# Attention, routed experts and a dense MLP on one core: two reorderings, in the attention loop and at the entry of the dense stage

## The chip, the cores and the metric

The kernel runs on one core of a Trainium2 chip. The core has a matrix engine (TensorE, PE in the profile, with its weight loads listed apart as PEld), a vector engine (VectorE, DVE), a scalar engine (ScalarE, ACT), a general engine (GpSimd, POOL) and a queue engine that only issues transfers (SyncE, SP). Each runs its own instruction stream in order, and they meet at semaphores. The metric is the device time of one execution in microseconds (us), the median over several.

## The reference

Three stages follow one another. Inputs and outputs are float32.

```python
# attention: 4 batches, 8 heads, 576 positions, head size 64; blockwise causal mask, blocks of 64
scores = q @ k.T / 8; scores = where(block_i >= block_j, scores, -1e9)
attn = exp(scores - max); attn = attn / (sum(attn) + 1e-9); out = attn @ v
x = out laid out as [2304 tokens, 512]

# routed experts: 8 experts of width 1024, one per token, tokens with x @ w_skip <= 0 pass unchanged
e = argmax(x @ w_gate); gate = softmax(x @ w_gate)[e]
x[active] = x + gate * (relu(x @ w1[e]) @ w2[e])

# dense MLP, width 2048
h = x @ w_in; g = max(h, 0) + alpha * min(h, 0); result = g @ w_out
```

## The kernel before, in words

**Attention** handles two heads at a time, a "pair": 16 pairs, numbered n. Pair 0 and pair 15 stand apart, pairs 1 to 14 are seven turns of a hardware loop with two pairs each. The 576 query rows of each head are cut into four tiles of 128 and a tail of 64; the two tails of a pair share one tile. So a pair has nine score units, c = 0 to 8: units 0 to 3 are the first head's tiles with 128, 256, 384 and 512 keys, units 4 to 7 the second head's, and unit 8 is the joint unit (JOINT) with both tails and 576 keys.

One unit passes through this chain: `scores` on PE (L640, JOINT L634, ending with a mask matmul L642), `maxima` on DVE (L981), `exps` on ACT (L849, followed by an accumulator read; `p_done` rises when both are done), `probs_t` on PE (transposes of the probabilities, L652), `pt_out` on DVE (copies them to SBUF, L992 and L989). Score units share three PSUM banks (0, 1, 2), so a score unit waits until the exps of the unit last in its bank are done: unit 1 of the next pair and unit 8 use bank 1, and unit 8 follows unit 6 there.

For the pair behind, n-1, three more pieces of work are placed among the units by number: `probs_v` (the value block, PE L662 and L668) at PV_AT, its evacuation `o_out` on ACT (L854, L856) at O_AT, `to_rows` (the row block, PE L685: it turns the output to token rows and adds the routing logits in the same matmuls) at ROWS_AT, and on DVE `x_out`, `x_tail_out` and `logits_part` (L1016 to L1041), which write the rows. For the pair ahead, n+1, five q/k chunks are transposed on PE (`qk_chunk`, L612 and L616) and evacuated on ACT (`qk_next`, L835 to L840) one unit later, at the units in QK_AT. Chunks and probability transposes use three PSUM banks in turn, in the order of ORDER, so each waits for the evacuation three places back. The lists before:

```python
QK_AT = [1, 2, 3, 5, 7]
PV_AT, O_AT, ROWS_AT, SUMS_AT = 0, 2, 2, 1
```

Every score unit is issued two units ahead of its transposes. SP runs one in-order queue per pair (`load_step`): load q and k of pair n+2 when the split of the pair before is done, load v of pair n when the value block of n-1 is done, `swap` (four transfers of q_t between partition halves, the first two once chunks 0 and 1 are evacuated, the next two after chunk 3; unit 0 of the next pair waits for the first two), two stores of zeros, and in pairs 1 to 8 two weight loads. POOL splits q and k into a rounded part and a rest.

**Experts.** Tokens are scattered by expert with indirect transfers (POOL L524), run through the two products in tiles of 128, and the results stored to `y_slots`.

**Dense MLP.** Six steps (c) of 384 tokens, three token tiles each. POOL gathers the three tiles' expert results (`gather`, L560), DVE adds them, times the gate, to the residual (`u_rows`, L1206), PE transposes by feature block (`u_transposes`, L781), ACT rounds (`u_out`, L946) and DVE takes the rest (`u_parts`, L1212), each for one feature block of 384 tokens through two banks. Then `hidden` (L793) and `project` (L804) follow for 16 blocks f of the width. In the first step all this stands in front of the first matmul; in later steps it lies beside work. Before the first gather POOL waits for the last store and runs a tiny operation on one column (L552). After the first gather POOL loads and splits w_out beside the first step.

## Time and profile before

| | |
|---|---|
| runs of the kernel before | 936.2, 937.68, 938.81 us; median 937.68 us |
| profiled execution | 941.46 us, of which the span is 939.6 us |
| busy share of the span | PE 89%, PEld 77%, DVE 46%, ACT 28%, POOL 26% |
| attention | from 15.8 us (first score unit) to 268.6 us (last row block) |
| router and scatter | to about 307 us |
| experts | to about 497 us |
| dense MLP | from 516.15 us (first product) to the end |
| granted TensorE clock | 0.96 of full in 24 to 285 us, 0.53 in 497 to 516 us, 1.00 from 585 us |

Matmul records overlap, since they include the time in which a matmul fills and drains the array, and their ends are modelled; the weight-load row (PEld) shows when the next matmul's weights go in. A wait is printed in brackets behind the row it held up, with the instruction that ended it. In the listings of waits, the columns are who waited, for whom, the sum in us, how many times, and the longest.

### The profile page before, as it was taken

The numbers are of one execution on the slowest core, as the hardware profiler recorded it, in microseconds if no ns is written. First come the engines' busy times: TensorE is split into PE (matmuls) and PEld (weight loads), VectorE is DVE, ScalarE is ACT, GpSimd is POOL, SyncE is SP. The second block draws the span as 40 slices with busy tenths as digits, with TensorE's granted clock in tenths as the row PEclk, the third lists the DMA queues.
The fourth block names the chain that finished last, engine by engine and source line by source line (L and its number), as shares of the span: only waits on it lengthen the run. The fifth ranks groups of instructions, "written<-read, shape, count | busy, mean of one in ns | idle before, by whom it ended". The sixth has DMA issues, their size and how long they took to land.

```text
span 939.6 us, 15516 instructions
## 1 busy us (share of the span) xinstructions
PE 832.4 (89%) x5243; PEld 723.7 (77%) x5244; DVE 432.3 (46%) x895; ACT 262.4 (28%) x643; POOL 243.4 (26%) x194
## 2 busy tenths in 40 slices
PE   4799999999930789999991999999999999999997
PEld 4577777777720688999981988998988998998996
DVE  2466566667671251232434464344353443443432
ACT  3355555556540221211321111111111112112111
POOL 4422333423007373330266891000001001000000
PEclk8899999999985798999996899999999999999999
DMA  4389899776304493541853320100100101100001
GB/s 113 71 228 244 244 229 260 173 193 166 115 7 184 165 369 114 184 174 45 302 211 90 101 68 0 67 0 12 56 0 17 50 0 28 39 0 12 23 1 33
DMA packets 97620, 103.06 MB, mean 110 GB/s; under 512 B 64320, under 2 KB 64320, under 8 KB 97088
## 3 DMA queue, kind: packets, MB, share of 16 engines
q1 hardware_dynamic: 89984, 74.50, 27.9%
q0 software_dynamic: 4448, 15.73, 5.6%
q10 hardware_dynamic: 3168, 12.58, 3.6%
q8 instruction: 11, 0.18, 0.1%
q14 instruction: 9, 0.07, 0.0%
HBM read 64.78 MB, written 27.53 MB: 98 GB/s over the span
## 4 chain that ended last, share of the span: by engine, by line
PE 71%; DVE 7%; POOL 6%; issue 6%; DMA 5%; SPq 3%; ACT 1%; DVEq 1%; ACTq 0%; POOLq 0%
PE bank L793 21%; PE bank L804 21%; PE bank L751 6%; PE bank L765 6%; PE bank L662 4%; PE bank L652 3%; PE bank L640 2%; PE bank L634 2%; PE bank L685 2%; POOL x_slots L524 2%; DVE neg_max L981 2%; DMA stage<-in_moe_w_in_dram 1%; DMA w_sb<-in_moe_w_dram 1%; POOL wi_lo L537 1%; PE bank L781 1%
## 5 line engine op out<-in xcount | busy, mean ns | idle before, releaser
L1220 DVE TENSOR_SCALAR g_sb<-bank,alpha_sb 128x384 f32<-128x384 f32 x96 | 59.3, 618 | 217.8 <-PE bank L793 217.3
L952 ACT CAST g_hi<-g_sb 128x384 fp32r<-128x384 f32 x96 | 49.5, 515 | 321.6 <-DVE g_sb L1222 321.6
L793 PE MATMUL bank<-u_hi,wi_hi 128*128 128x384 f32 x384 | 130.5, 340 | 1.2 <-DVE u_lo L1212 1.2
L793 PE MATMUL bank<-u_hi,wi_lo 128*128 128x384 f32 x384 | 130.5, 340 | 0.0
L793 PE MATMUL bank<-u_lo,wi_hi 128*128 128x384 f32 x384 | 130.0, 339 | 0.0
L804 PE MATMUL bank<-wo_lo,g_hi 128*128 128x512 f32 x288 | 113.8, 395 | 0.0
L804 PE MATMUL bank<-wo_hi,g_lo 128*128 128x512 f32 x288 | 113.5, 394 | 0.0
L804 PE MATMUL bank<-wo_hi,g_hi 128*128 128x512 f32 x288 | 112.7, 391 | 0.6 <-DVE g_lo L1226 0.6
L751 PEld LDWEIGHTS bank<-rows_t,w_sb 128*128 128x128 f32 x832 | 96.9, 195 | 2.6 <-DVE rows_t L1151 1.5
L751 PE MATMUL bank<-rows_t,w_sb 128*128 128x128 f32 x832 | 97.2, 279 | 1.1 <-DVE rows_t L1151 1.1
L849 ACT ACTIVATE p_sb<-bank,neg_max 128x128 f32<-128x128 f32 (+2 forms) x144 | 79.7, 554 | 61.7 <-DVE neg_max L981 61.5
L981 DVE TENSOR_REDUCE neg_max<-bank 128x1 f32<-128x128 f32 (+2 forms) x144 | 73.7, 512 | 41.1 <-PE bank L634 19.7
L992 DVE COPY p_t<-bank 128x128 f32<-128x128 f32 (+3 forms) x128 | 60.8, 476 | 50.6 <-PE bank L652 50.6
L640 PE MATMUL bank<-k_t,q_t 128*128 128x128 f32 (+3 forms) x256 | 71.3, 365 | 11.4 <-DMA alpha_sb<-in_moe_alpha_dram 5.3
L793 PEld LDWEIGHTS bank<-u_hi,wi_hi 128*128 128x128 f32 x384 | 73.1, 190 | 5.2 <-DVE u_lo L1212 1.6
L652 PE MATMUL bank<-ident,p_sb 128*128 128x128 f32 x400 | 73.4, 289 | 4.1 <-DVE p_t L992 2.1
L560 POOL DMA_INDIRECT u_sb<-y_slots,from_i x18 | 19.1, 1059 | 221.9 <-PE bank L781 217.8
L793 PEld LDWEIGHTS bank<-u_lo,wi_hi 128*128 128x128 f32 x384 | 72.9, 190 | 3.6
L793 PEld LDWEIGHTS bank<-u_hi,wi_lo 128*128 128x128 f32 x384 | 72.9, 190 | 0.0
L492 POOL TENSOR_TENSOR parts<-qk_nat,zero_c 128x512 fp32r<-128x512 f32 (+1 forms) x30 | 33.7, 1145 | 146.4 <-DMA qk_nat<-in_k_dram 146.4
L804 PEld LDWEIGHTS bank<-wo_lo,g_hi 128*128 128x128 f32 x288 | 54.0, 188 | 11.6
L804 PEld LDWEIGHTS bank<-wo_hi,g_hi 128*128 128x128 f32 x288 | 54.1, 188 | 10.2 <-issue 1.2
(143 smaller groups left out, 1286.2 us busy)
## 6 DMA issues: line engine op xcount, KB each, us to landing
w_sb<-in_moe_w_dram ACTq DMA_DIRECT2D x6, 2048.0 KB, 7.9
w_sb<-in_moe_w_dram SPq DMA_DIRECT2D x6, 2048.0 KB, 9.2
q_t<-q_t SPq DMA_DIRECT2D x64, 160.0 KB, 2.5
w_sb<-in_moe_w_dram SPq DMA_DIRECT2D x16, 512.0 KB, 6.3
x_slots<-x_tok SPq DMA_DIRECT2D x14, 512.0 KB, 3.3
y_slots<-x_tok SPq DMA_DIRECT2D x14, 512.0 KB, 4.9
qk_nat<-in_q_dram SPq DMA_DIRECT2D x32, 128.0 KB, 4.4
qk_nat<-in_k_dram SPq DMA_DIRECT2D x32, 128.0 KB, 3.0
```

Source lines behind the costliest of these rows:

```text
L640: pe.matmul(a[:, 0:keys], q_t[:, par, z, h, P * (i + 1):P * (i + 2)], k_t[:, par, h, 0:keys], start=z == 0, stop=False)
L652: last = pe.transpose(t[:, P * j:P * j + P], p_sb[:, c % PB, P * j:P * j + P], ident[:])
L662: last = pe.matmul(O_MAIN[HALF * h:HALF * h + HALF, P * unit:MAIN], v_nat[:, unit, h, :], p_t[:, h, unit, P * unit:MAIN], start=unit == 0, ...
L751: last = pe.matmul(HIDDEN[c][:, P * z:P * z + P], w1_sb[:, par, j, P * f:P * f + P], rows_t[:, j, :], start=j == 0, stop=j == KD - 1)
L765: last = pe.matmul(RESULT, h[:, f, :], w, start=f == 0 and z == 0, stop=f == KF - 1 and z == 2)
L793: last = pe.matmul(dst, w[:, j, P * f:P * f + P], u[:, j, :], start=z == 0, stop=z == len(terms) - 1)
L804: last = pe.matmul(YBANK[i][:, :], g[:, f % GB, P * i:P * i + P], w[:, f, :], start=f == 0 and z == 0, stop=f == FI - 1 and z == 2)
L849: act.activation(p_sb[:, c % PB, 0:keys], scores_ap(c), ACT.Exp, bias=neg_max[:, c:c + 1], accum_out=row_sum[:, par, i, h:h + 1]).then_inc ...
L952: act.copy(g_hi[:, f % GB, :], g_sb[:, f % 2, :]).then_inc(g_hi_done, 1)
L981: dve.reduce_max(neg_max[:, c:c + 1], scores_ap(c), AX.X, negate=True).then_inc(max_done, 1)
L992: dve.tensor_copy(p_t[:, h, 0:i + 1, P * i:P * i + P], t[:, 0:P * (i + 1)].rearrange("p (j c) -> p j c", c=P)).then_inc(pt_evac, 1)
L1220: dve.tensor_scalar(g, a, 0.0, alpha_sb[:, f:f + 1], ALU.min, ALU.mult).then_inc(neg_done, 1)
```

## The change

In attention, the row block moves from unit 2 to the front of unit 8 (JOINT), on PE and on DVE. Score unit 3 moves from unit 1 to unit 0, in front of the value block, so that unit 0 issues two score units and unit 1 none. The q/k chunks move: chunk 0 from unit 1 to 2, chunk 1 from 2 to 3, chunk 4 from 7 to 6. The sums move from unit 1 to 0. The row block's banks are now read by DVE until shortly before the next value block writes them, so `probs_v` gets a wait on `head_part_done`, which starts at one.

At the entry of the dense stage, the first chunk is handled by token tile: each gathered tile has its own semaphore, DVE adds it as soon as it is there, PE transposes its four feature blocks into a bank of its own, and ACT and DVE evacuate that bank whole. The wait for the input weights' split now stands behind the transposes. The tiny POOL operation becomes a semaphore increment.

```diff
-        QK_AT = [1, 2, 3, 5, 7]
-        PV_AT, O_AT, ROWS_AT, SUMS_AT = 0, 2, 2, 1
+        QK_AT = [2, 3, 3, 5, 6]
+        PV_AT, O_AT, SUMS_AT, ROWS_AT = 0, 2, 0, JOINT
+        AHEAD = {c: [c + 2] for c in range(UNITS)}
+        AHEAD[PV_AT], AHEAD[PV_AT + 1] = [2, 3], []
+        UFIRST = [bank[1], bank[2], bank[5]]
...
-            pool.tensor_tensor(zero_c[:], zero_c[:], zero_c[:], ALU.add).then_inc(all_stored, 1)
+            pool.sem_inc(all_stored, 1)
...
-                                            ).then_inc(gathered, 16)
+                                            ).then_inc(gathered if c else first_gathered[i], 16)
...
                 pe.wait_ge(pt_evac, UNITS * n + JOINT)
+                pe.wait_ge(head_part_done, n + 1)
...
             def pair(n, par, first=False, last=False):            # PE
                 for c in range(UNITS):
-                    if c + 2 < UNITS:
-                        scores(c + 2, n, par, first)
-                    elif not last:
-                        scores(c + 2 - UNITS, n + 1, 1 - par, False)
+                    if c == ROWS_AT and not first:
+                        to_rows(n - 1)
+                    for u in AHEAD[c]:
+                        if u < UNITS:
+                            scores(u, n, par, first)
+                        elif not last:
+                            scores(u - UNITS, n + 1, 1 - par, False)
                     if c == PV_AT and not first:
                         probs_v(n - 1)
-                    if c == ROWS_AT and not first:
-                        to_rows(n - 1)
                     probs_t(c, n, last)
...
+            def first_transposes():
+                for i in range(CH):
+                    pe.wait_ge(u_ready, i + 1)
+                    for j in range(KD):
+                        last = pe.transpose(UFIRST[i][:, P * j:P * j + P], u_sb[:, i, P * j:P * j + P], ident[:])
+                    last.then_inc(u_tr, 1)
...
+            first_transposes()
             pe.wait_ge(wi_split, KD)
-            u_transposes(0)
...
             def pair(n, par, first=False, last=False):            # DVE
                 for c in range(UNITS):
+                    if c == ROWS_AT and not first:
+                        x_out(n - 1)
+                        x_tail_out(n - 1)
+                        logits_part(n - 1)
...
-                    if c == ROWS_AT and not first:
-                        x_out(n - 1)
-                    if c == ROWS_AT + 1 and not first:
-                        x_tail_out(n - 1)
-                        logits_part(n - 1)
...
+            dve.sem_inc(head_part_done, 1)
...
+            def first_row(i):
+                dve.wait_ge(first_gathered[i], 16)
+                dve.scalar_tensor_tensor(u_sb[:, i, :], u_sb[:, i, :], gate[:, i:i + 1], x_tok[:, i, :], ALU.mult, ALU.add
+                                         ).then_inc(u_ready, 1)
+            def first_part(i):
+                dve.wait_ge(u_hi_done, i + 1)
+                dve.tensor_tensor(u_lo[:, :, P * i:P * i + P], UFIRST[i][:].rearrange("p (j n) -> p j n", j=KD),
+                                  u_hi[:, :, P * i:P * i + P].bitcast(F32), ALU.subtract).then_inc(u_lo_done, 1)
...
-            u_rows(0)
-            u_parts(0)
+            first_row(0)
+            first_row(1)
+            first_part(0)
+            first_row(2)
+            first_part(1)
+            first_part(2)
```

ACT's `first_out` copies each of the three banks to `u_hi` the same way, and the semaphore counts of the later steps are shifted to match.

TensorE in the loop, from the score unit behind JOINT's to the next: L640 (now L645) are score units, L652 (now L657) transposes of probabilities, L616 a q/k chunk, L685 (now L691) the row block. Before:

```order
L623 ISA
L629 ISA
L640 MATMUL bank<-k_t,q_t 128x128 x2
L642 MATMUL bank<-mask_r,mask_l 128x64
L650 REGISTER_ALU
L652 MATMUL bank_4<-ident,p_sb 128x128 x4
L603 REGISTER_ALU
L616 MATMUL bank<-ident,parts 128x128 x4
L640 MATMUL bank_2<-k_t,q_t 128x256 x2
L642 MATMUL bank_2<-mask_r,mask_l 128x64
L650 REGISTER_ALU
L652 MATMUL bank_4<-ident,p_sb 128x128 x5
```

After:

```order
L647 MATMUL bank<-mask_r,mask_l 128x64
L608 REGISTER_ALU
L655 REGISTER_ALU
L657 MATMUL bank<-ident,p_sb 128x128 x4
L680 ISA
L691 ISA
L691 MATMUL bank<-w_route,o_t 128x146 x5
L645 MATMUL bank_2<-k_t,q_t 128x256 x2
L647 MATMUL bank_2<-mask_r,mask_l 128x64
L608 REGISTER_ALU
L655 REGISTER_ALU
L657 MATMUL bank_4<-ident,p_sb 128x128 x5
```

The chunk is gone from between unit 7's transposes and score unit 1 of the next pair (128x256), and the row block stands there instead.

ScalarE in the loop from the exponentials of unit 3 to those of unit 5: L849 (now L864) are exponentials, L835 to L840 (now L850 to L855) evacuate q/k chunks. Before:

```order
L838 ACTIVATE q_t<-bank_4 128x512
L845 REGISTER_ALU
L849 ACTIVATE p_sb,row_sum<-bank,neg_max 128x512
L831 REGISTER_ALU
L835 ACTIVATE q_t<-bank_4 128x2x64
L836 CAST k_t<-bank_4 128x2x64
L845 REGISTER_ALU
L849 ACTIVATE p_sb,row_sum<-bank_2,neg_max 128x128
L831 REGISTER_ALU
L840 CAST k_t<-bank 128x512
L845 REGISTER_ALU
L849 ACTIVATE p_sb,row_sum<-bank_2,neg_max 128x256
```

After:

```order
L864 ACTIVATE p_sb,row_sum<-bank,neg_max 128x512
L846 ISA
L853 ACTIVATE q_t<-bank 128x512
L860 REGISTER_ALU
L864 ACTIVATE p_sb,row_sum<-bank_2,neg_max 128x128
L846 REGISTER_ALU
L850 ACTIVATE q_t<-bank_4 128x2x64
L851 CAST k_t<-bank_4 128x2x64
L846 REGISTER_ALU
L855 CAST k_t<-bank 128x512
L860 REGISTER_ALU
L864 ACTIVATE p_sb,row_sum<-bank_2,neg_max 128x256
```

The first three chunks stood in front of unit 3, between 3 and 4, and between 4 and 5. Now the first stands between 3 and 4, and the other two together between 4 and 5.

VectorE at the entry of the dense stage: u_sb are the rows, u_lo the rests. Before:

```order
L1189 CAST wi_hi<-wi_raw 128x2048
L1192 TENSOR_TENSOR wi_lo<-wi_raw,wi_hi 128x2048 x2
L1206 SCALAR_TENSOR_TENSOR u_sb<-u_sb,gate,x_tok 128x512 x3
L1212 TENSOR_TENSOR u_lo<-bank_4,u_hi 128x384 x4
L1242 UNCONDITIONAL_BRANCH
```

After:

```order
L1211 CAST wi_hi<-wi_raw 128x2048
L1214 TENSOR_TENSOR wi_lo<-wi_raw,wi_hi 128x2048 x2
L1220 SCALAR_TENSOR_TENSOR u_sb<-u_sb,gate,x_tok 128x512 x2
L1225 TENSOR_TENSOR u_lo<-bank_2,u_hi 128x4x128
L1220 SCALAR_TENSOR_TENSOR u_sb<-u_sb,gate,x_tok 128x512
L1225 TENSOR_TENSOR u_lo<-bank_2,u_hi 128x4x128
L1225 TENSOR_TENSOR u_lo<-bank,u_hi 128x4x128
```

The first rest is taken before the third tile's rows, and each rest spans one token tile and four feature blocks.

## Rows read from the trace of the kernel before

**Rows 1.** Waits of the weight loader in attention, 18 to 285 us.

```profile
PEld bank L634 <- ACT p_sb L849: 10.3, 15, 1.3
...
PEld bank L640 <- ACT p_sb L849: 6.3, 14, 0.5
...
PEld bank L652 <- ACT p_sb L849: 2.9, 14, 0.2
PEld bank L652 <- DVE p_t L992: 2.2, 3, 1.4
```

**Rows 2.** One pair's timeline, TensorE: start us, length us, engine, line, what, [idle, releaser].

```profile
204.77 0.20 PEld L662 LDWEIGHTS bank<-p_t,v_nat 128*64 128x64 f32 x4
...
209.21 1.30 PEld L685 LDWEIGHTS bank<-w_route,o_t 128*128 128x128 f32 x10
...
214.89 1.32 PEld L634 LDWEIGHTS bank<-k_t,q_t 128*128 128x128 f32 x8 [0.64 <-ACT p_sb L849]
214.89 1.55 PE L634 MATMUL bank<-k_t,q_t 128*128 128x512 f32 x8 [0.40 <-ACT p_sb L849]
...
216.53 0.30 PEld L640 LDWEIGHTS bank<-k_t,q_t 128*128 128x128 f32 x2
...
218.16 0.30 PEld L640 LDWEIGHTS bank<-k_t,q_t 128*128 128x128 f32 x2 [0.47 <-ACT p_sb L849]
```

**Rows 3.** The same timeline, ScalarE.

```profile
211.32 0.28 ACT L835 ACTIVATE q_t<-bank 128x128 fp32r<-128x128 f32 x1 [0.82 <-PE bank L612]
...
212.51 0.59 ACT L840 CAST k_t<-bank 128x512 fp32r<-128x512 f32 x1 [0.40 <-PE bank L616]
...
212.99 0.48 ACT L849 ACTIVATE p_sb<-bank,neg_max 128x256 f32<-128x256 f32 x1
...
214.16 0.58 ACT L849 ACTIVATE p_sb<-bank,neg_max 128x384 f32<-128x384 f32 x1 [0.60 <-DVE neg_max L981]
...
214.64 0.19 ACT L849 ACTIVATION_READ_ACCUMULATOR p_sb<-bank,neg_max 128x1 f32 x1
```

**Rows 4.** The same timeline, VectorE.

```profile
211.57 0.56 DVE L1016 TENSOR_TENSOR x_tok<-bank,inv_sum 128x384 f32 x1
...
213.37 0.29 DVE L1041 TENSOR_TENSOR head_part<-bank,inv_sum 128x54 f32 x2
213.59 0.54 DVE L981 TENSOR_REDUCE neg_max<-bank 128x1 f32<-128x384 f32 x1
```

**Rows 5.** Busy time by stretch: length, PE, PEld, DVE, ACT, POOL, clock, DMA share, GB/s.

```profile
124.20:139.30 15.10, 14.30 (x121) 11.30 (x121) 9.92 (x28) 8.68 (x28) 4.76 (x4) 1.00 0.93 237
...
199.84:214.89 15.05, 14.30 (x122) 11.30 (x122) 9.83 (x29) 8.63 (x27) 5.13 (x5) 1.00 0.66 172
```

**Rows 6.** The same timeline as rows 2, SP's swap transfers.

```profile
212.03 4.61 SPq L362 DMA_DIRECT2D q_t<-q_t  x4
```

**Rows 7.** The 64 swap transfers, from issue to landing.

```profile
DMA to landing us min/median/max: 2.4/2.5/4.3
```

**Rows 8.** Timeline of VectorE before the dense stage.

```profile
496.28 4.49 DVE L1192 TENSOR_TENSOR wi_lo<-wi_raw,wi_hi 128x2048 fp32r<-128x2048 f32 x2
508.40 2.86 DVE L1206 SCALAR_TENSOR_TENSOR u_sb<-u_sb,gate,x_tok 128x512 f32<-128x512 f32 x3 [7.63 <-DMA u_sb<-y_slots,from_i]
```

**Rows 9.** Timeline of GpSimd, same place.

```profile
497.52 1.11 POOL L552 TENSOR_TENSOR zero_c<-zero_c 128x1 f32<-128x1 f32 x1 [9.31 <-DMA y_slots<-y_sb]
498.90 2.79 POOL L560 DMA_INDIRECT u_sb<-y_slots,from_i  x1 [0.28 <-POOL zero_c L552]
502.00 0.95 POOL L560 DMA_INDIRECT u_sb<-y_slots,from_i  x1 [0.30 <-issue]
```

**Rows 10.** Chain that ended last, at the scatter: start us, us, what.

```profile
281.27 2.85 POOL x_slots L524
```

**Rows 11.** Timeline of TensorE, same place as rows 8.

```profile
511.41 1.51 PE L781 MATMUL bank<-ident,u_sb 128*128 128x128 f32 x6 [17.21 <-DVE u_sb L1206]
...
516.15 0.69 PE L793 MATMUL bank<-u_hi,wi_hi 128*128 128x384 f32 x1 [1.16 <-DVE u_lo L1212]
```

More of the change, by code:

```diff
@@ L229, in program @@
         gathered = sem("gathered")
+        first_gathered = [sem(f"first_gathered{i}") for i in range(CH)]
         u_ready = sem("u_ready")
@@ L557, in gather @@
                 if c:
-                    pool.wait_ge(u_tr, KD * c)
+                    pool.wait_ge(u_tr, CH + KD * (c - 1))
                 for i in range(CH):
@@ L689, in pair @@
                 for c in range(UNITS):
-                    if c + 2 < UNITS:
-                        scores(c + 2, n, par, first)
-                    elif not last:
-                        scores(c + 2 - UNITS, n + 1, 1 - par, False)
+                    if c == ROWS_AT and not first:
[5 more added lines that the diff above has]
+                            scores(u - UNITS, n + 1, 1 - par, False)
                     if c == PV_AT and not first:
                         probs_v(n - 1)
-                    if c == ROWS_AT and not first:
-                        to_rows(n - 1)
                     probs_t(c, n, last)
-                    if c in QK_AT and not last:
-                        j = QK_AT.index(c)
-                        if j == 0:
-                            pe.wait_ge(split_done, n + 2)
-                        qk_chunk(j, 1 - par, ring("qk", j, n, last))
+                    for j, at in enumerate(QK_AT):
+                        if at == c and not last:
+                            if j == 0:
+                                pe.wait_ge(split_done, n + 2)
+                            qk_chunk(j, 1 - par, ring("qk", j, n, last))
             pe.wait_ge(const_ready, 1)
@@ L772, in _ @@
                 tiles(2 * e2 + 1, 1, e2)
+            def first_transposes():
[4 more added lines that the diff above has]
+                    last.then_inc(u_tr, 1)
             def u_transposes(c):
[L776 removed]
+                pe.wait_ge(u_ready, CH + c)
                 for j in range(KD):
                     if j >= 2:
[L779 removed]
+                        pe.wait_ge(u_lo_done, CH + KD * (c - 1) + j - 1)
                     for i in range(CH):
@@ L789, in hidden @@
                 if f == 0:
-                    pe.wait_ge(u_lo_done, KD * c + KD)
+                    pe.wait_ge(u_lo_done, CH + KD * c)
                 terms = [(w, u, j) for j in range(KD) for w, u in ((wi_hi, u_hi), (wi_hi, u_lo), (wi_lo, u_hi))]
@@ L865, in pair @@
                         o_out(n - 1)
-                    if c - 1 in QK_AT and not last:
-                        qk_next(QK_AT.index(c - 1), n, par)
+                    for j, at in enumerate(QK_AT):
+                        if at == c - 1 and not last:
+                            qk_next(j, n, par)
             act.wait_ge(const_ready, 1)
@@ L940, in _, with first_out @@
             act.copy(wi_hi[:, KD - 1, :], wi_raw[:, KD - 1 - LATE, :]).then_inc(late_hi, 1)
+            def first_out():
+                for i in range(CH):
+                    act.wait_ge(u_tr, i + 1)
+                    act.copy(u_hi[:, :, P * i:P * i + P], UFIRST[i][:].rearrange("p (j n) -> p j n", j=KD)).then_inc(u_hi_done, 1)
             def u_out(c):
                 for j in range(KD):
-                    act.wait_ge(u_tr, KD * c + j + 1)
+                    act.wait_ge(u_tr, CH + KD * (c - 1) + j + 1)
                     act.copy(u_hi[:, j, :], UBANK[j % 2][:, 0:CT]).then_inc(u_hi_done, 1)
@@ L969, in _ @@
             act.sem_inc(out_stored, 16)
-            u_out(0)
+            first_out()
             with act.Fori(0, T_TILES // CH - 1) as c:
@@ L1052, in pair @@
                 for c in range(UNITS):
-                    if c + 2 < UNITS:
-                        maxima(c + 2, n)
-                    elif not last:
-                        maxima(c + 2 - UNITS, n + 1)
+                    if c == ROWS_AT and not first:
+                        x_out(n - 1)
+                        x_tail_out(n - 1)
+                        logits_part(n - 1)
+                    for u in AHEAD[c]:
+                        if u < UNITS:
+                            maxima(u, n)
+                        elif not last:
+                            maxima(u - UNITS, n + 1)
                     if c == SUMS_AT and not first:
```

8 lines of the change are left out of this document (3 added, 5 removed).

## The prediction

> **What bounds the kernel.** I read the busy shares first (PE 89%, the others far below), then the chain that ended last, then the waits of PE in each stage, then one pair's timeline on all engines. In attention, TensorE is the engine that everything else follows, but it does not run without a break. The weight loader waits there for exponentials 43 times, 19.5 us, and three times for VectorE's copies, 2.2 us: 21.7 us in all [rows 1]. Three of these waits come back in every pair: 0.64 us before the joint unit's scores (they need unit 6's exponentials), 0.47 us before unit 1 of the next pair (it needs the joint unit's), and about 0.2 us before unit 5's transposes [rows 1, 2]. A pair takes 15.05 us [rows 5], so without them it would take 13.75.
>
> How much such a wait costs is itself a choice. The record of the joint unit's first matmul shows an idle time of 0.40 us, its weight load 0.64 us [rows 2]. The matmul records include the time to drain, and in a stream without waits the next weight load starts before they end, so I count the weight loader's gap. The Trainium skill (Perfetto Trace Analysis, Identifying the Most-Contended Engine) says the same: matmul busy time is a bad measure, the weight loads' is a good one. By matmul records the waits would be worth only some 12 us.
>
> At the entry of the dense stage TensorE stands still from the last expert tile to 516.15 us, but for twelve transposes. There the chain is what counts: last gather, rows, transposes, rounding, rests.
>
> **Attention, wait by wait.** I set time zero at the value block's first weight load, 204.77 us [rows 2]. The work on TensorE is the same; only the order differs.
>
> *Unit 1 of the next pair.* Before, it came 0.47 us too early [rows 2]. Now the row block stands in front of it (1.30 us of weight loads, [rows 2]), while chunk 4 has been moved ahead. ScalarE evacuates chunk 4 before it takes the joint unit's exponentials, which moves these about 0.5 us later. 1.30 less 0.5 is more than 0.47 by 0.3, so the wait goes, with little to spare.
>
> *Joint unit.* Before, unit 6's maximum started at 213.59 us, right behind the last of the rows' steps on VectorE (213.37 and 0.29 more), and its exponentials started when it was done [rows 3, 4]. That work has moved away, so the maximum starts as soon as unit 6's scores are there, some 0.3 to 0.6 us earlier. What comes last next is ScalarE itself: between the end of chunk 0 on TensorE and the joint unit, it has chunk 0, unit 4, chunk 1, chunk 2, unit 5 and unit 6 to do. By the lengths 0.59, 0.28 twice, 0.59, 0.57 and 0.67 [rows 3], with 0.47 taken for unit 4 and about 0.1 of overlap at each joint (212.51 plus 0.59 against a next start at 212.99), that is 3.1 to 3.2 us. TensorE has in the same stretch what it had before from the row block's end (209.21 + 1.30 = 210.51) to 214.89, 4.38 us, less the waits of 0.84 and less three transposes of unit 2 (0.34 by my reading of the pitch): 3.2 us. About 0.3 of this passes before chunk 0's records end. So ScalarE is late by 0.2 to 0.3 us, spread over unit 5's transposes and the joint unit. I take 0.25 us for each of 14 pairs: 3.5 us. Between its bounds (no wait, or a handover more per chunk, 0.8 us) this is nearest to the rows.
>
> *The new wait of the value block.* VectorE's four row results take 0.56 to 0.27 us each ([rows 4], first and last of them), 1.4 us in all and about 1.2 with their overlap. They start when the row block's records end, and TensorE has unit 1's scores, five transposes and two score units to do meanwhile, over 2 us. It costs nothing, with some 0.5 us of cover. Behind it on TensorE everything would be held up. VectorE's next maximum (unit 1) and the joint copy come about 1.2 us later; TensorE needs the first only behind the value block, 3 us later, and the second for the value block's tail.
>
> *The swap transfers.* Before, the first two were issued at 212.03 us [rows 6], 7.26 after zero. With 0.6 us to the second and 2.5 us to landing [rows 7] they were there at 10.4, and unit 0 of the next pair came at 11.76 (216.53, [rows 2]). Now chunk 1 is evacuated at about 6.0, the transfers issue at about 6.3 and land at 9.4, and unit 0 comes at about 9.8. The slack falls from 1.4 to 0.4 us. In pairs 1 to 8 the transfer engines are 93% busy, against 66% later [rows 5], and SP reaches the swaps later, since loading q, k, v and weights fills its queue. I take 0.3 us of wait for each of the eight, 2.4 us, between 0 and the whole gain.
>
> *The last pair* has no chunks. Its wait for VectorE before the joint transposes (the longest, 1.4 us, [rows 1]) is covered by the row block, its joint unit waits less (about 0.5 us left), but the last value block now waits for the row results, which have only five transposes in front of them: 1.0 us. Left over: 1.5 us. Pair 0 ends in a wait for small loads; I count nothing there, and take 0.5 us out of the 21.7.
>
> Sum: 21.2 - 3.5 - 2.4 - 1.5 = 13.8 us.
>
> **The entry of the dense stage.** Before: the three tiles were there at 508.40 us, the first product started at 516.15, 7.75 us later [rows 8, 11]. Now, behind the last tile: one row step (0.95, a third of 2.86, [rows 8]), four transposes (two thirds of the 1.51 us that six took, [rows 11]), one rounding of 512 columns (0.59, as for a chunk, [rows 3]), one rest (0.75, estimated by the same width) and handovers of 0.3: 3.6 us. Tiles 0 and 1 come 1.5 us and more earlier, one after another, and are through before. Gain 4.1 us.
>
> The gathers start earlier too. The tiny POOL operation took 1.11 us and the first gather 2.79, against 0.95 for the next one; both ended 0.1 and 0.9 us after one of VectorE's two splits (496.28 to 500.77, [rows 8, 9]). The same shows at the scatter, 2.85 us beside a split [rows 10]. So an indirect transfer's issue waits until VectorE's two-input operation ends. Without the tiny operation the first gather gets in at 498.6, the second at 500.8, and the third is issued 1.25 us earlier. Gain 1.2 us. The Trainium skill (SBUF — State Buffer, Who interferes with whom) says that a tensor_tensor does not stall descriptor writing, only GpSimd's reads; the rows show the stall all the same. By that rule the gain would be the tiny operation's 1.4 us, nearly the same.
>
> The clock of the first products stays low as before (0.69 us for the first, [rows 11]), since TensorE has been idle just as long. Dense gain: 5.3 us, between 3 (rows held up by GpSimd's w_out splits) and 6.5. After that TensorE is busy, w_out's splits are far ahead, and the rest shifts.
>
> **Sum.** 13.8 + 5.3 = 19.1 us, from 941.46 to 922.4 for the profiled execution. The timed median before is 937.68, 3.8 us lower; with the same difference 918.6 us.
>
> **Rivals.**
> 1. *Transfers set pairs 1 to 8.* For: 93% busy at 15.05 us per pair [rows 5]; the same bytes in 14.0 us leave no air. Against: q and k are loaded two pairs ahead. Then 8 times 0.75 us is not gained: 924.6 us.
> 2. *Two chunks in a row on ScalarE.* The joint unit waits 0.8 us instead of 0.25 in 14 pairs. For: the evacuation of chunk 0 ends just when chunk 2 needs its bank. Against: ScalarE is idle a third of a pair. 926.3 us. About the same would come out if matmul records were the right measure.
> 3. *The third tile's rows come behind GpSimd's first split of w_out*, which took 1.6 us: it would cost about 1.6 us, 920.2 us. The Trainium skill (same page and section) has whichever starts first block the other for its whole length; the rows show only the mixed 2.86 us for three.
> 4. *Slower: the swap sets the pair.* From the swap's landing over unit 0, the row block, the value block (7.0 us), SP's loads of v (2.3) and the issue (0.9) there are 10.2 us plus the landing time. With 2.5 us this is 12.7 and hidden. It decides from 3.8 us on, and the change loses from 4.9 us on. The longest landing was 4.3 us [rows 7]. If it rose to 6.2 in 13 pairs, each would take 1.35 us more than before: 17.5 lost, 6 to 7 kept: 948 us.
>
> **How the numbers follow.** Likeliest case 0.60, rival 1 0.15, rival 2 0.12, rival 3 0.09, rival 4 0.04. If every wait went and the entry gave 6.5, it would be 912. The range is 912.5 to 929. A difference under 0.3% (2.8 us) can't be told from none. Every case but the fourth is clearly faster; a mixture of rivals 1 and 2 with a poor entry could come near no change. Faster 0.92, same 0.04, slower 0.04.
>
> **What would show it.** A pair of about 14.0 us late in attention and 14.3 early; no wait before unit 1 of the next pair; a wait of 0.2 to 0.3 us before unit 5's transposes or the joint unit, ended by exponentials; none on the row results but in the last pair; the first product of the dense stage 3.6 us after the third tile. A wait on swapped q_t in most pairs, or a late pair above 14.6 us, would prove me wrong.

## The result and the profile after

The changed kernel takes 916.56 us (median of 4, 915.13 to 918.93), the kernel before beside it 938.05 (4 runs, 936.2 to 938.81): a ratio of 0.9763, 95% interval 0.9738 to 0.9788. The profiled execution has a span of 917.1 us against 939.6. Forecast were 918.6 us and a gain of 19.1; measured are 21.5 by the medians and 22.5 by the spans.

The page of the changed kernel, busy time and the slices of TensorE and the transfers:

```profile
PE 824.1 (90%) x5243; PEld 724.6 (79%) x5244; DVE 431.3 (47%) x894; ACT 264.6 (29%) x642; POOL 241.0 (26%) x193
...
PE   5799999999802979999986999999999999999997
...
PEclk9899999999955989999996999999999999999999
DMA  5499999775225755532943312002002002000001
```

TensorE does the same work (its share rises because the span is shorter). Where the time went is read by stages. Times from the two traces' timelines, TensorE's weight loads:

| stretch | before, us | after, us | change | forecast |
|---|---|---|---|---|
| start to the first scores behind the small loads | 35.56 | 32.99 | -2.6 | 0 |
| from there to pair 15's value block | 228.25 | 212.14 | -16.1 | -13.8 |
| from there to the last expert's copy | 230.61 | 232.52 | +1.9 | 0 |
| last expert's copy to the dense stage's first product | 21.73 | 15.88 | -5.9 | -5.3 |
| from there to the end of the span | 423.4 | 423.6 | +0.1 | 0 |

**Attention.** The waits of TensorE from 18 to 285 us (us in total, times, longest), to be set against [rows 1]:

```profile
PE bank L645 <- DMA alpha_sb<-in_moe_alpha_dram: 3.6, 1, 3.6
PEld bank L657 <- ACT p_sb L864: 2.8, 14, 0.2
PE bank L645 <- DMA q_t<-q_t: 2.5, 5, 0.7
...
PEld bank L645 <- ACT p_sb L864: 1.0, 1, 1.0
PE bank L668 <- DVE head_part L1062: 0.9, 1, 0.9
...
PEld bank L639 <- ACT p_sb L864: 0.3, 1, 0.3
```

The wait before the joint unit (15 times, 10.3 us) is left once, 0.3 us, in the last pair; that before unit 1 (14 times, 6.3) is left once, 1.0 us, in pair 0. The third, 0.20 us before unit 5's transposes, has stayed in every pair. New are 2.5 us, five times, for swapped q. One late pair, weight loads (start, length, engine, line, what, [idle, releaser]); [rows 2] answers:

```profile
199.73 1.32 PEld L639 LDWEIGHTS bank<-k_t,q_t 128*128 128x128 f32 x8
...
202.12 0.42 PEld L657 LDWEIGHTS bank<-ident,p_sb 128*128 128x128 f32 x4
202.51 1.29 PEld L691 LDWEIGHTS bank<-w_route,o_t 128*128 128x128 f32 x10
203.74 0.31 PEld L645 LDWEIGHTS bank<-k_t,q_t 128*128 128x128 f32 x2
...
204.11 0.53 PEld L657 LDWEIGHTS bank<-ident,p_sb 128*128 128x128 f32 x5
...
205.08 0.31 PEld L645 LDWEIGHTS bank<-k_t,q_t 128*128 128x128 f32 x2
...
205.82 0.23 PEld L668 LDWEIGHTS bank<-p_t,v_nat 128*64 128x64 f32 x4
...
212.85 0.20 PEld L657 LDWEIGHTS bank<-ident,p_sb 128*128 128x128 f32 x2 [0.20 <-ACT p_sb L864]
...
213.46 1.32 PEld L639 LDWEIGHTS bank<-k_t,q_t 128*128 128x128 f32 x8
```

From joint unit to joint unit it is 13.73 us, against 15.05 before. The row block (L691) stands between unit 7's transposes (202.12) and unit 1's scores of the next pair (203.74). What these need, the joint unit's exponentials, ended at 203.45, 0.3 us earlier, and VectorE's row results at 205.70, 0.12 us ahead of the value block's first weights at 205.82:

```profile
202.61 0.75 ACT L864 ACTIVATE p_sb<-bank,neg_max 128x576 f32<-128x576 f32 x1
...
203.25 0.20 ACT L864 ACTIVATION_READ_ACCUMULATOR p_sb<-bank,neg_max 128x1 f32 x1
...
204.53 0.56 DVE L1037 TENSOR_TENSOR x_tok<-bank,inv_sum 128x384 f32 x1 [1.02 <-PE bank L691]
...
205.40 0.30 DVE L1062 TENSOR_TENSOR head_part<-bank,inv_sum 128x54 f32 x2
```

In pairs 1 to 8, joint unit 1 to joint unit 9, a pair takes 14.27 us. Length, TensorE, weight loads, VectorE, ScalarE, GpSimd, clock, DMA share, GB/s; the transfer engines, 93% busy in [rows 5], are full:

```profile
44.25:158.41 114.16, 110.78 (x971) 91.21 (x969) 80.50 (x218) 70.69 (x208) 35.51 (x29) 1.00 0.98 255
199.73:213.46 13.73, 13.64 (x124) 11.37 (x123) 9.99 (x29) 8.79 (x26) 4.64 (x5) 1.00 0.72 189
```

**Entry of the dense stage.** Last difference of w_in, gathers, then the third tile on its way:

```profile
479.50 4.49 DVE L1214 TENSOR_TENSOR wi_lo<-wi_raw,wi_hi 128x2048 fp32r<-128x2048 f32 x2
481.61 1.10 POOL L565 DMA_INDIRECT u_sb<-y_slots,from_i  x1 [10.18 <-POOLq L557]
483.01 1.81 POOL L565 DMA_INDIRECT u_sb<-y_slots,from_i  x1 [0.30 <-issue]
485.13 0.95 POOL L565 DMA_INDIRECT u_sb<-y_slots,from_i  x1 [0.30 <-issue]
...
490.20 0.75 DVE L1220 SCALAR_TENSOR_TENSOR u_sb<-u_sb,gate,x_tok 128x512 f32<-128x512 f32 x1 [1.17 <-DMA u_sb<-y_slots,from_i]
...
490.92 1.04 POOL L576 TENSOR_TENSOR wo_hi<-y_out,zero_c 128x512 fp32r<-128x512 f32 x1 [3.15 <-DMA y_out<-in_moe_w_out_dram]
...
491.01 1.12 PE L787 MATMUL bank<-ident,u_sb 128*128 128x128 f32 x4 [1.41 <-DVE u_sb L1220]
...
492.17 0.59 ACT L962 CAST u_hi<-bank 128x512 fp32r<-128x512 f32 x1 [1.94 <-PE bank L787]
492.78 0.69 DVE L1225 TENSOR_TENSOR u_lo<-bank,u_hi 128x512 fp32r<-128x512 f32 x1 [1.23 <-ACT u_hi L962]
...
493.53 0.69 PE L808 MATMUL bank<-u_hi,wi_hi 128*128 128x384 f32 x1 [1.40 <-DVE u_lo L1225]
```

[rows 8, 9, 11] answer to these. The gathers are issued by 486.08, 8.43 us behind the last expert's copy (477.65); before it was 504.20, 9.78 behind (494.42). From there to the first product 7.45 us instead of 11.95. So in these two traces 1.35 us come from the gathers and 4.5 from the tiles' separate ways. The traces taken below show that 15.88 us from the last copy to the first product is the shortest: eleven with the new entry lie between 15.88 and 16.83, mean 16.2, and the two with the old one at 21.7. Taken so, the entry is worth 5.5 us. The third tile's row step begins at 490.20, ahead of GpSimd's split of w_out at 490.92, and the first product follows 3.33 us later.

### The profile page after: what moved, and what is told of

Its sections match the earlier page's. It is cut to its first block, busy times and chain, and to the rows that moved or that the text cites. A ratio compares the mean times of both kernels' runs of the same rounds, so it can differ in the third digit from the quotient of the medians.

```text
span 917.1 us, 15528 instructions
## 1 busy us (share of the span) xinstructions
PE 824.1 (90%) x5243; PEld 724.6 (79%) x5244; DVE 431.3 (47%) x894; ACT 264.6 (29%) x642; POOL 241.0 (26%) x193
## 4 chain that ended last, share of the span: by engine, by line
PE 74%; DMA 6%; SPq 6%; POOL 5%; issue 3%; DVE 3%; ACT 2%; ACTq 0%; DVEq 0%; POOLq 0%
PE bank L808 22%; PE bank L819 21%; PE bank L758 7%; PE bank L772 7%; PE bank L657 4%; PE bank L668 3%; PE bank L645 3%; DMA w_sb<-in_moe_w_dram 3%; POOL x_slots L529 2%; PE bank L621 2%; PE bank L691 2%; DMA q_t<-q_t 1%; POOL w_lo L552 1%; SPq L343 1%; PE bank L639 1%
## 5 line engine op out<-in xcount | busy, mean ns | idle before, releaser
L864 ACT ACTIVATE p_sb<-bank,neg_max 128x128 f32<-128x128 f32 (+2 forms) x144 | 79.2, 552 | 59.1 <-DVE neg_max L1002 56.6
L645 PE MATMUL bank<-k_t,q_t 128*128 128x128 f32 (+3 forms) x256 | 70.7, 370 | 9.7 <-DMA q_t<-q_t 5.2
L657 PE MATMUL bank<-ident,p_sb 128*128 128x128 f32 x400 | 70.1, 287 | 1.8 <-DVE p_t L1013 0.3
L1013 DVE COPY p_t<-bank 128x128 f32<-128x128 f32 (+3 forms) x128 | 60.6, 484 | 17.7 <-PE bank L657 16.5
```

The source lines that it names most:

```text
L645: pe.matmul(a[:, 0:keys], q_t[:, par, z, h, P * (i + 1):P * (i + 2)], k_t[:, par, h, 0:keys], start=z == 0, stop=False)
L657: last = pe.transpose(t[:, P * j:P * j + P], p_sb[:, c % PB, P * j:P * j + P], ident[:])
L864: act.activation(p_sb[:, c % PB, 0:keys], scores_ap(c), ACT.Exp, bias=neg_max[:, c:c + 1], accum_out=row_sum[:, par, i, h:h + 1]).then_inc ...
L1013: dve.tensor_copy(p_t[:, h, 0:i + 1, P * i:P * i + P], t[:, 0:P * (i + 1)].rearrange("p (j c) -> p j c", c=P)).then_inc(pt_evac, 1)
```

## Experiments

Each was timed in five rounds beside the kernel before, unless it is called a single run. "J" is the start of a pair's joint unit.

### The two parts apart

*attention_only* has the attention part of the diff and none of the dense part, *dense_only* the reverse.

> Only the attention part of the change: chunks placed later, row block ahead of the joint unit, units 2 and 3 scored ahead of the value block. The dense entry stays as before. Theory (read from the two traces): pair 0 and the small loads give 2.6 us, pairs 1 to 15 give 16.1, the expert stage gives 1.9 back, the dense entry stays at 21.7 us from the last expert's copy to the first product. Sum 16.8: 938.0 - 16.8 = 921.2 us. By the terms of my forecast (13.8) it would be 924.2. Rival: the expert stage's 1.9 belongs to one execution and not to the change; then 919.3.

> Only the dense part: no tiny POOL operation, first chunk's tiles gathered, added, transposed and rounded one by one. Attention as before. Theory: 5.85 us from the dense entry alone, 938.0 - 5.9 = 932.1 us; attention and experts as in the kernel before (first scores behind the small loads at 35.6 us, expert stage 230.6 us from the last value block to the last copy). Rival: the entry gains only beside a changed attention, or the 2.6 us of pair 0 are chance: then the first scores behind the small loads come near 33 us here too, and the total is near 929.5.

Measured: 921.45 us (ratio 0.9818, 0.9793 to 0.9843) and 934.13 us (0.9947, 0.9928 to 0.9966), beside 938.94. The gains are 17.5 and 4.8 us (by the ratios 17.1 and 5.0); together 22.3, against 21.5 to 22.6 for the whole change in two sets. They add up. The theories had 921.2 and 932.1 us; the dense part alone gave a little less than the 5.85 of its theory, which is near the 5.5 above. From the last copy to the first product it is 21.68 us with the attention part alone and 16.06 with the dense part alone: the gain of this stretch belongs to the dense part. Both rivals touch the stretches outside, and the traces speak to both. The stretch from the scatter's first transfer to the last expert's copy was 214.6 us before, 216.5 after, 212.7 here and 217.6 here; so the 1.9 us of the table do not follow the attention part. The first scores behind the small loads come at 33.58 us in *dense_only* though its attention is the old one, so not all of the 2.6 us need be the change's.

### The row block back

```diff
-        PV_AT, O_AT, SUMS_AT, ROWS_AT = 0, 2, 0, JOINT
+        PV_AT, O_AT, SUMS_AT, ROWS_AT = 0, 2, 0, 2
```
On TensorE the block stands behind unit 4's scores again, on VectorE the row results behind unit 2's and 3's copies.

> The changed kernel with the row block and VectorE's row results back at unit 2, behind unit 4's scores; chunks and the order of score units stay new. Theory: the row block is what filled the wait before unit 1 of the next pair. That unit then comes 0.5 to 1.0 us before the joint unit's exponentials are done (they are 0.5 later through chunk 4), and VectorE's rows again delay later maxima, 0.2 to 0.6 us before the joint unit. In 14 pairs 10 to 20 us: about 931 us, no earlier than 927. Rival: the scores of unit 3 ahead and the later chunks gave the gain, the row block's place little: 917 to 920 us.

Measured: 933.16 us (0.9932, 0.9909 to 0.9956). A late pair takes 14.95 us. Its weight loads:

```profile
212.91 1.33 PEld L639 LDWEIGHTS bank<-k_t,q_t 128*128 128x128 f32 x8 [0.21 <-ACT p_sb L864]
...
216.67 0.30 PEld L645 LDWEIGHTS bank<-k_t,q_t 128*128 128x128 f32 x2 [0.96 <-ACT p_sb L864]
```

The wait before unit 1 of the next pair is now 0.96 us, twice the old 0.47 [rows 2], as expected from chunk 4 standing ahead of the joint unit's exponentials; before the joint unit 0.21. The theory holds, the rival falls: without the row block at its new place, the other two edits are worth 0.1 us per pair.

### The chunks back

```diff
-        QK_AT = [2, 3, 3, 5, 6]
+        QK_AT = [1, 2, 3, 5, 7]
```

> The changed kernel with the q/k chunks back at units 1, 2, 3, 5 and 7; the rest stays new. Theory: the chunks' place decides little, since ScalarE has room elsewhere: a late pair within 0.3 us of 13.72; in pairs 1 to 8 the swaps are issued some 1 us earlier, and the 2.5 us of waits on q_t shrink. 914 to 919 us. Rival: chunks 0 to 2 late are what keeps ScalarE in time for the joint unit; then the wait before the joint unit is back at 0.5 us or more in each pair and the time is 924 us or above.

Measured: 924.47 us (0.9848, 0.9825 to 0.9872). A late pair takes 14.18 us, 0.46 more, so my theory falls; but the rival named the wrong place. There is no wait before the joint unit in the loop. It is before unit 3's transposes (L657), and ScalarE shows why:

```profile
215.62 0.60 ACT L853 ACTIVATE q_t<-bank 128x512 fp32r<-128x512 f32 x1 [0.70 <-PE bank L621]
...
216.11 0.68 ACT L864 ACTIVATE p_sb<-bank,neg_max 128x512 f32<-128x512 f32 x1
...
216.94 0.42 PEld L657 LDWEIGHTS bank<-ident,p_sb 128*128 128x128 f32 x4 [0.39 <-ACT p_sb L864]
```

ScalarE has idled 0.70 us for chunk 0, which now comes from unit 1, and only then takes unit 3's exponentials (216.11), which could have run since the value block. TensorE waits 0.39 us for them. With chunk 0 at unit 2, unit 3's exponentials go first (209.16 us in the changed kernel), and the same transposes start without a wait at 210.39.

### Unit 3's scores back, and the row block alone

```diff
-        AHEAD[PV_AT], AHEAD[PV_AT + 1] = [2, 3], []
```
*scores_back* leaves out this line, so that unit 3 is scored behind the value block. *rows_alone* leaves it out and has the old chunks too: of the attention part only the row block's move is left.

> The changed kernel with unit 3's scores back behind the value block (unit 1's scores in the joint step, unit 2's ahead of the value block, unit 3's behind it); row block and chunks stay new. Theory: unit 3's scores are cover. Without them TensorE comes to the value block about 0.6 us earlier, and there waits for VectorE's row results or for the joint unit's copy, and unit 3's exponentials start after the value block instead of during it, so the transposes of unit 3 wait too. 0.4 to 1.0 us more in each of 14 pairs: 922 to 931 us, and a late pair of 14.1 to 14.7 us. Rival: there was cover enough, a late pair stays within 0.15 us of 13.72 and the time is 915 to 919 us.

> The changed kernel with only the row block moved: chunks and score units stand as before the change (row block ahead of the joint step's scores, value block waits for the row results). Theory: the row block fills the wait before unit 1, worth 0.5 us; but TensorE is then at the value block before VectorE's row results are through (0.6 to 0.9 us, as with unit 3's scores back) and unit 3's transposes wait for exponentials. A late pair of 14.7 to 15.1 us, 927 to 933 us. Rival: the row block alone brings more than half of the gain: a late pair below 14.4 us and a time below 924.

Measured: 926.66 us (0.9865, 0.9837 to 0.9892) and 930.64 us (0.9903, 0.9878 to 0.9929), late pairs of 14.50 and 14.73 us. Both theories hold. Their waits for the row results, TensorE, 18 to 264 us:

```profile
PE bank L667 <- DVE head_part L1061: 8.8, 15, 0.9
```

```profile
PE bank L667 <- DVE head_part L1061: 8.7, 15, 0.8
...
PEld bank L656 <- ACT p_sb L863: 7.3, 28, 0.3
```

0.6 us in each pair stand at the value block, where the changed kernel has none. The cover that unit 3's scores give was needed, and without it the row block's move costs that much. The six orders of the attention, by the length of a late pair: none of the edits 15.05, row block alone 14.73, chunks and scores 14.95, row block and chunks 14.50, row block and scores 14.18, all three 13.72. The edits do not add: alone the row block gives 0.32 us, as the last of three 1.23.

### The transfers of pairs 1 to 8

```diff
-                    sp.dma_start(w2_sb[:, par, bass.ds(W2Q * m - W2Q, W2Q), :], ...)
+            with sp.Fori(1, KD + 1) as m:
+                load_step(m + 2 * KD)
+                for par in range(2):
+                    sp.dma_start(w2_sb[:, par, bass.ds(W2Q * m - W2Q, W2Q), :], ...)
```

> The changed kernel; the loads of w1 for the first two experts stay in pairs 1 to 8, those of w2 move to pairs 9 to 12, two to a pair. Pairs 1 to 8 then move a 0.5 MB piece less each. Theory (transfers): the 4.4 us that pairs 1 to 8 take longer than eight late pairs (14.27 against 13.72 each), with waits of the scores for swapped q, come from transfer engines that are 93% busy; they fall to 1 to 2 us, pairs 9 to 12 grow by 0 to 0.2 us each: 913 to 915 us. Rival (the issuing queue: SP's own issues ahead of the swaps, whose number the edit hardly changes): pairs 1 to 8 stay near 14.27 and the time near 916.5.

Measured: 913.87 us (0.9726, 0.9700 to 0.9752). From J1 to J9 eight pairs take 109.78 us, 13.72 each: no excess over eight late pairs, against 4.40 us in the changed kernel (114.16). Then pairs 9 to 12, with two pieces each, take 13.73, 14.74, 14.01 and 14.35 and give 1.95 back:

```profile
42.61:152.39 109.78, 109.06 (x971) 90.98 (x970) 79.94 (x218) 70.28 (x208) 36.24 (x30) 1.00 0.90 227
166.12:209.22 43.10, 41.68 (x366) 34.22 (x365) 30.26 (x83) 26.51 (x78) 15.35 (x13) 1.00 0.99 257
```

The rival's forecast (near 14.27 and 916.5) missed. But its cause is not excluded, since the edit takes two things out of each early pair at once: 0.5 MB, and one of the 17 issues of SP's in-order queue, which took 0.9 us itself (median of the eight).

The traces show which step is late. These are SP's swaps in an early and in a late pair of the changed kernel; the joint units behind them start at 58.02 and 199.73 us:

```profile
57.75 2.71 SPq L367 DMA_DIRECT2D q_t<-q_t  x4
```

```profile
198.30 3.65 SPq L367 DMA_DIRECT2D q_t<-q_t  x4
```

| kernel, joint unit | first swap issued ahead of it, us | the pair that starts with it, us |
|---|---|---|
| changed kernel, late pairs | 1.43 to 1.44 | 13.72 |
| changed kernel, J2 to J5 | 0.27, 0.83, 0.40, 1.04 | 14.66, 14.08, 14.51, 13.88 |
| changed kernel, J6 to J9 | 0.27, 0.63, 0.61, 1.04 | 14.66, 14.29, 14.31, 13.88 |
| weights_spread, J10 to J12 | 0.18, 0.90, 0.57 | 14.74, 14.01, 14.35 |

Where the lead is under 1.2 us, the pair is longer by just what it lacks of 1.2; with more lead it is not longer. Once issued, the swaps land as fast as ever: 2.4 us (median, longest 2.8) in the eight early pairs at 0.98 of the transfer engines, 2.4 (longest 2.7) in the late ones. So TensorE waits because SP comes late to the swap, and not because the swap's own transfers are slow. Ahead of its swaps SP still waited for chunks 12 times, 8.8 us, in the eight early pairs of *weights_spread*, but only 4 times, 2.1 us, in those of the changed kernel: its queue has hardly any time left there. What fills it, the number and length of its issues or full engines that make the issues longer (those of the k loads took 2.6 us a pair against 2.2 in *weights_spread*), stays open: no run moves the bytes and leaves the issue, or the reverse. The payback in pairs 9 to 12 is larger than expected (1.95 us, against at most 0.8).

### The small loads

```diff
-            pe.wait_ge(small_loaded, 80)
...
                 pe.wait_ge(o_evac, 2 * n + 2)
+                pe.wait_ge(small_loaded, 80)
                 hp = n % HP
```

> The changed kernel; TensorE waits for the small loads (routing weights, alpha) not behind pair 0 but where they are first used, at the row block in pair 1's joint step. Theory: since the row block has moved there, nothing needs them earlier; the wait of 3.6 us goes, with 0.5 us of it left in waits for exponentials: 916.6 - 3 = 913.5 us, and the joint units of pairs 0 and 1 stand 16.5 to 17 us apart instead of 19.8. Rival: pair 1 then waits for its q, k splits or swaps as long: no change, 916.5.

Measured: 913.15 us (0.9707, 0.9681 to 0.9734), span 912.0. J0 to J1 is 13.42 us instead of 19.77: 6.35 us for a wait of 3.6. The rest is TensorE's clock. The stretch behind the wait in the changed kernel, and one that holds most of the same work without the wait (columns as above):

```profile
33.00:38.00 5.00, 5.00 (x14) 2.21 (x16) 1.74 (x6) 0.67 (x2) 0.00 (x0) 0.50 0.43 95
```

```profile
28.00:32.00 4.00, 3.94 (x26) 2.44 (x28) 2.87 (x9) 1.59 (x7) 1.09 (x1) 1.00 0.17 8
```

The granted clock fell while TensorE stood still; it is 0.50 (1.2 GHz) for the 5 us that start with the first scores, and 1.00 (2.4 GHz) from 39 us on. Without the wait it does not fall. From unit 2's scores to the value block's tail (L674) TensorE takes 5.76 us behind the wait and 3.28 without it, so the wait costs some 2.5 us more than its length; that is what the forecast of 16.5 to 17 us between the joint units had left out. Before the change it was the same (0.50 from 35.6 to 40.6 us). But J1 to J9 takes 115.48, 1.32 more than in the changed kernel: waits for swapped q (six, 3.7 us, against five, 2.5) take part of it back. By the spans 5.1 us are left, by the medians 3.4, by the ratios to the kernel before 5.3.

### Both, and the changed kernel again

*both* has the small loads' wait at the row block and these loads:

```diff
+            with sp.Fori(1, KD + 1) as m:
+                load_step(m + 2 * KD)
+                w2_piece(0, m)
+            load_step(3 * KD + 1)
+            w2_piece(1, 1)
             load_step(PAIRS - 2)
+            w2_piece(1, 2)
+            w2_piece(1, 3)
             sp.wait_ge(pv_done, 2 * (PAIRS - 1))
             load_v(PAIRS - 1)
+            w2_piece(1, 4)
```

> The changed kernel with both later versions together: TensorE waits for the small loads at the row block, and the first two experts' w2 pieces go one to a pair in pairs 9 to 13, two in pair 14, the last in pair 15 (with weights_spread two went into each of pairs 9 to 12, and these lost 2 us in all). Theory: transfers bound a pair only where two 0.5 MB pieces stand in it beside q, k, v, swaps and zeros. Then all pairs but the last are 13.7 us, 4.4 us less than the changed kernel; the small loads give 3.4; sum 7.8: 908.8 us, between 907 and 911. Rival: the gains overlap (the early pairs, freed of one wait, wait for transfers instead, as the longest of small_later's did with 15.0 us): 911 to 913.

> The changed kernel once more, unchanged. Theory: its time is 916.6 us within 1.5. Its trace repeats what belongs to the change (late pairs 13.72 us, dense entry 15.9 us) and differs in what belongs to one execution: the stretch from the scatter's first transfer to the last expert's copy, which was 216.5 us in the changed kernel and 214.6 before, may lie anywhere from 212 to 218. Rival: that stretch is 216.5 again within 0.5 us, so that its 1.9 us belong to the change.

Measured, in the same set: 907.43 us (0.9653, 0.9628 to 0.9678) and 916.31 us (0.9752, 0.9729 to 0.9774). *both* beats the changed kernel by 8.9 us: the theory's 907 to 911 holds, the rival's 911 to 913 does not. From J2 on all its pairs take 13.70 to 13.73 us, and the last 12.91. Only J1 to J2 is long (14.95; its swaps are issued 0.01 us ahead of the joint unit), so J1 to J9 has 1.19 us too many; the transfer engines are 0.89 busy there and 0.92 from J10 to J13:

```profile
38.22:149.17 110.95, 109.31 (x971) 91.06 (x970) 79.94 (x218) 70.37 (x208) 40.81 (x34) 1.00 0.89 226
162.89:204.05 41.16, 40.90 (x366) 34.14 (x364) 29.95 (x83) 26.35 (x78) 14.88 (x13) 1.00 0.92 228
```

*changed_again* has late pairs of 13.72 us, an excess of 4.7 us in pairs 1 to 8 (4.4 before) and 16.03 us at the dense entry. Its scatter to last copy took 215.88 us, 0.6 less than the first time, which does not decide between its two theories. All the traces together do: in the fourteen of this case that stretch lies between 212.7 and 217.6 us, 214.6 and 217.6 with the old attention, 212.7 to 216.5 with the whole new one. The 1.9 us are not the change's.

### What holds the gathers

Before, and with the attention part alone, the first gather follows the tiny operation and takes 2.79 us beside VectorE's difference of w_in:

```profile
476.40 4.49 DVE L1199 TENSOR_TENSOR wi_lo<-wi_raw,wi_hi 128x2048 fp32r<-128x2048 f32 x2
...
477.64 1.10 POOL L555 TENSOR_TENSOR zero_c<-zero_c 128x1 f32<-128x1 f32 x1 [9.31 <-DMA y_slots<-y_sb]
479.03 2.79 POOL L563 DMA_INDIRECT u_sb<-y_slots,from_i  x1 [0.28 <-POOL zero_c L555]
```

Two single runs change VectorE's work there:

```diff
-                dve.tensor_tensor(wi_lo[:, t, :], wi_raw[:, t - LATE, :], wi_hi[:, t, :].bitcast(F32), ALU.subtract
+                dve.tensor_copy(wi_lo[:, t, :], wi_raw[:, t - LATE, :]).then_inc(wi_split, 1)
```
```diff
+                dve.tensor_tensor(wi_lo[:, t, :], wi_raw[:, t - LATE, :], bank[1][:, 0:1].to_broadcast([P, FD]), ALU.subtract
```

> The changed kernel with VectorE's late differences of w_in (two inputs in SBUF) replaced by plain copies of the same size (the subtraction is left out; the results of the dense stage are not meant to be used). Theory: it is the two-input operation that holds back an indirect transfer's issue; beside plain copies each gather takes 0.95 to 1.15 us, where the second now takes 1.81, and the third gather starts up to 0.9 us earlier. Rival: any VectorE operation on SBUF of that size holds it: a gather beside a copy takes 1.8 us or more again. The last copy of the experts to the first product: 15.0 to 15.9 us either way.

> The changed kernel; VectorE's two late differences of w_in read their second input from PSUM and so only one from SBUF (the numbers are not the reference's; length and output size stay). The copies of the run before, 1.23 us each, held a gather back too, so two inputs are not the condition. Theory: what holds the gathers is VectorE's use of a second SBUF port, for a second input or for a fast copy; with one input at this slow pace no gather waits: 1.10, 0.95 and 0.95 us. Rival: any VectorE operation that reads and writes SBUF holds them: 1.8 us or more for one of the gathers.

Measured with copies, 915.43 us:

```profile
477.53 1.23 DVE L1214 CAST wi_lo<-wi_raw 128x2048 fp32r<-128x2048 f32 x1 [0.70 <-ACT wi_hi L956]
477.71 1.96 POOL L565 DMA_INDIRECT u_sb<-y_slots,from_i  x1 [10.19 <-POOLq L557]
```

and with the second input in PSUM, 914.64 us:

```profile
475.74 4.49 DVE L1214 TENSOR_TENSOR wi_lo<-wi_raw,bank 128x2048 fp32r<-128x2048 f32 x2
477.85 1.04 POOL L565 DMA_INDIRECT u_sb<-y_slots,from_i  x1 [12.58 <-POOLq L557]
479.19 0.96 POOL L565 DMA_INDIRECT u_sb<-y_slots,from_i  x1 [0.31 <-issue]
480.45 0.95 POOL L565 DMA_INDIRECT u_sb<-y_slots,from_i  x1 [0.30 <-issue]
```

The first theory falls: a copy has one input and holds a gather too, which ended 0.91 us after the copy's end (478.76). Operations of the old length (4.49 us for two) with one input from SBUF hold none: two gathers run beside them at their full pace. So what counts is neither VectorE being busy nor the two inputs as such; the reading that both a second SBUF input and a fast copy take a way that the gather's issue needs fits all three kernels, but which part of the issue needs it no run shows. The last copy to the first product took 15.91 us with copies and 15.29 so, against 15.88.

## Why the prediction was right, step by step

**Which record counts a wait.** Right. Two of the three gaps of the weight loader, 0.64 and 0.47 us [rows 2], are gone from every late pair, and the pair is 1.33 us shorter. The matmul records would have given 0.40 and 0.2. The rest of the 1.33, some 0.2 us, is nothing that I named. It lies between the weight loads of unit 1's scores and the transposes behind them: 0.57 us in each late pair before, 0.37 after (203.74 to 204.11 above). No listed wait stands there, and no run shows what shortened it. The value block is as long as before (2.89 and 2.91 us).

**ScalarE's lateness, 3.5 us.** Nearly right. I counted the old 0.20 us as gone and put 0.25 of new lateness into each pair; what is there is 0.20 before unit 5's transposes, 2.8 us in all. A late pair is 13.72 us and not 14.0 mainly because of the 0.2 us that I had not named. At the joint unit itself lateness appears only with the row block back (0.21), and with chunk 0 early it stands at unit 3 (0.39).

**The wait for the row results.** Right in both places: none in the loop, 0.9 us in the last pair (forecast 1.0). But the cover is 0.12 us and not the 0.5 that I gave it. That the cover is unit 3's scores, which the forecast only listed among others, was shown by taking them away: 0.6 us per pair.

**The swaps in pairs 1 to 8, 2.4 us.** The mechanism was right, that SP reaches the swaps later because loads fill its queue, and its size too small: 4.4 us, and 4.7 in the repeat. Rival 1 had said 6 us, by the bytes; *weights_spread* brought the excess to zero, but by taking out an issue together with the bytes, so it does not decide for them. A pair of 14.27 us is the 14.3 that I had named by luck, because the late pair under it was 0.28 us shorter than forecast.

**The last pair, 1.5 us.** 0.9 and 0.3 us by the waits, 1.2.

**Pair 0 and the small loads, 0.** Here the first of the table's rows gave 2.6 us. The wait ends with the small loads, which SP issues behind the swaps of pair 1. In the kernels with the old places of the chunks (before, *dense_only*, *chunks_back*, *rows_alone*) TensorE goes on at 35.56, 33.58, 34.57 and 34.20 us; in eight traces with the new ones between 31.52 and 33.80, mean 32.65. So some 1.8 us go with the chunks' places and the rest with the one execution. About 0.9 of it is the end of those swaps; the other 0.9 is one issue among the small loads, which took 1.2 to 2.3 us in those four kernels and 0.6 in seven of the eight. Why the chunks' places should do this no run shows. I had put nothing there because the stretch ends in a wait; I had not asked what starts the transfer that it waits for.

**The dense entry, 5.3 us.** In the two traces 4.1 for the tiles was 4.5 and 1.2 for the gathers was 1.35, and by the mean of all traces the whole is 5.5; the last tile took 3.33 us where I had worked out 3.6.

**The sum.** 18.7 us of attention instead of 13.8, 5.85 instead of 5.3, and 1.9 back in the expert stage, which is the spread of that stage. The time was met more closely than the terms, which is in part luck: the unnamed 0.2 us a pair (some 3 us) and pair 0's 1.8 were missed on one side, the swaps' 2.0 and the expert stage's 1.9 on the other. One sum was wrong: with no wait left and 6.5 us at the entry the gain is 21.2 + 6.5, which gives 910 us and not 912, so the range's fast end stood 2 us too high. Rivals 2 and 3 (two chunks in a row, the third tile behind the split) did not appear, rival 4 neither.

## What to carry to other kernels

When a block is moved into a wait, look for the cover of what is then late: here the row block was worth 0.32 us of a pair alone and 1.23 with the chunks and one score unit moved as well, so edits that are tested one at a time would have looked poor. When a wait ends with a transfer, follow it back to the instruction ahead of the issue, and put the wait where the data is first used: after the row block's move the small loads' wait stood a pair too early, and its 3.6 us of standstill cost TensorE 2.5 more at the lower clock. Before shortening a loop, work out its transfers per turn against the new length, and also the queue that issues them: transfer engines 93% busy at 15.05 us were full at 14.3, the issuing queue had no time left either, and moving one piece out of each turn gave back the whole excess.

## What the runs showed of the hardware

- SP's in-order queue took about 0.9 us to issue one 0.5 MB weight load. A swap's transfers landed 2.4 us (median) after their issue at 0.98 of the transfer engines' time (255 GB/s of this mixture) as at lower shares; what grew was the delay of the issue, and pairs waited up to 0.7 us for swapped q. At 0.90 (227 GB/s) none did, at 0.89 in *both* one did, 0.9 us.
- An indirect transfer's issue on GpSimd (0.95 us) was held by a VectorE difference with both inputs in SBUF (2.79 and 1.81 us) and by a plain copy of 1.23 us (1.96), and not by a difference with one input in PSUM (1.04, 0.96, 0.95).
- The first of the gathers started 3.96 us behind the last expert's copy without the tiny GpSimd operation and 4.48 with it: of its 1.11 us only 0.5 were saved at that place; the rest of the 1.35 came from the gathers meeting the differences at another moment.
